# Issuing the attention stage's 24 output stores from SyncE instead of ScalarE

## The chip, the cores and the metric

The kernel runs on one core of a Trainium2 chip. The metric is the device time of one execution in microseconds (us), lower is better; of several executions the median counts.

## The reference

Chunked local attention with 8 memory keys, then two MLPs, one after the other, all in f32.

```python
q, k, v: (4, 8, 768, 64); mem_k, mem_v: (4, 8, 8, 64)     # batch, heads, tokens, head_dim
for c in range(768 // 32):                                # chunks of 32 tokens
    rows = slice(32 * c, 32 * c + 32)
    ctx  = slice(max(0, 32 * c - 16), min(768, 32 * c + 40))
    k_full, v_full = cat(mem_k, k[:, :, ctx]), cat(mem_v, v[:, :, ctx])
    a = softmax(q[:, :, rows] @ k_full.T / 8)
    attn[:, :, rows] = a @ v_full
x = attn.transpose(0, 2, 1, 3).reshape(3072, 512)
h = x @ w_in                                              # 512 x 2048
g = (a0 + a1*h + a2*h**2 + a3*h**3) / (1 + |b0|*|h| + |b1|*h**2 + 1e-6)
x = g @ w_out                                             # 2048 x 512
out = ((x @ w1) * (x @ w2)) @ w3 @ w_out2                 # 512 x 1024 twice, 1024 x 1024, 1024 x 512
```

## The kernel before

**Three stages.** The first stage, attention_and_weights, folds w3 and w_out2 into one matrix (until about 70 us of the trace), computes the attention, and splits most of the first MLP's weights into a high and a low part. The function mlps holds the two others: the first MLP, in 6 blocks of 512 tokens and 16 slots of the hidden width, and the second MLP, in 6 blocks and 8 slots. All products of the MLPs are made of three matmuls (high by high, high by low, low by high). Stage one and mlps are two blocks of the program, and no engine goes into the second before all of them have ended the first.

**The attention.** It walks over 24 tiles of 128 tokens, 6 to each batch (TPB = 6, TILES = 24); t is the number of the tile over all batches. For a tile TensorE transposes the normalised probabilities (L740), computes the scores of the tile three further on (L724, L731), transposes q and k of a later half batch in the first three batches (L712), and multiplies the probabilities by v (L753, called pv here). VectorE does the softmax (L597 to L626). ScalarE copies the transposed probabilities out of PSUM (L495), computes the exp of the tile two further on (L490), copies the product of pv out of bank 6 into one of the two buffers of xt_sb (copy_xT, L501), and then issues the DMA which stores that buffer into xT in DRAM (store_x, L507). In between it copies transposed q and k (L479, L481).

**What is ordered by hand.** Each engine runs its own list of instructions in order, and the lists are tied by semaphores. For the change these ties matter:

- copy_xT of tile t waits until the store of tile t - 2 has landed (xt_stored), since both use the same buffer;
- pv of tile t waits for its v tile, which has three buffers (v_loaded), and for copy_xT of tile t - 1 (xt_ready), since all tiles share bank 6;
- SyncE issues all loads. Its step of tile t (tile_step) issues in this order: two or three loads of q and k of a later half batch (where there is one, L297 and L304), the v loads of tile t + 3 (L326, L330), for which it waits until pv of tile t is done, and one load of a raw weight for GpSimd (L171 or L174), for which it waits until GpSimd has used the buffer before it;
- after the step of tile 15 SyncE loads the first 512 tokens of xT back as x_raw (L413). ScalarE splits off their high part after copy_xT of tiles 18 and 19 (x_his, L532), VectorE the low part after its work on tiles 19 and 20 (x_los, L668), and TensorE runs two products of the first MLP on them, inside tiles 22 and 23.

```python
            def tile_step(t):
                ...
                if t + V_BUFS < TILES:
                    sp.wait_ge(pv_done, t + 1)
                    load_v(*after(b, pos, V_BUFS))
                if t < LATE:
                    sp.wait_ge(raw_split, 2 * EARLY + t + 1)
                    load_raw(*sh.late(t + 2))
```

Of the kernel before, what the change touches and what calls it, by code (L numbers as in the profile page):

```python
# [34 lines left out]
P = 128  # L35
LINE = 1024
B, H, S, D = 4, 8, 768, 64
# [5 lines left out]
TPB = S // P  # L43
# [50 lines left out]
def after(b, pos, n=1):  # L94

    return b + (pos + n) // TPB, (pos + n) % TPB
# [116 lines left out]
def attention_and_weights(nc, q, k, v, mem_k, mem_v, w_in, w_out, w3, w_out2, poly_a, poly_b,  # L213
                          xT, bweights, weights, base, work, banks, bank, sh):
    with ExitStack() as ctx:  # L215
        x_raw, x_hi, x_lo, coef = sh.x_raw, sh.x_hi, sh.x_lo, sh.coef
        x_loaded, coef_loaded, x_hi_ready = sh.x_loaded, sh.coef_loaded, sh.x_hi_ready
        wf_stored, xt_stored = sh.wf_stored, sh.xt_stored
# [3 lines left out]
        def sem(name):  # L222
            return ctx.enter_context(nc.semaphore(name))
# [31 lines left out]
        xt_sb = Place(nc, sh.raw_at - 2 * BLK * 4, sh.raw_at)("xt_sb", [P, 2, KC, P])  # L255
# [16 lines left out]
        pv_done, xt_ready = sem("pv_done"), sem("xt_ready")  # L272
# [20 lines left out]
        def _(sp):  # L293
# [13 lines left out]
            def load_qk(hb, gs):  # L307

                for g in gs:
                    if g < Q_GROUPS:  # L310
                        if hb >= 2:
                            sp.wait_ge(turned, 1 + TURNED * (hb - 2) + PAIRS)
                        load_q(hb, g)
                    else:
                        if hb >= 2:
                            sp.wait_ge(turned, 1 + TURNED * (hb - 1))
                        load_k(hb, g - Q_GROUPS)

            def load_v(b, pos):
                u = pos % V_BUFS  # L320
                for w in range(2):
                    s = pos * P + w * WIN - LEFT
                    lo, hi = max(-s, 0), min(CTX, S - s)
                    for r0, r1 in ((lo, min(hi, CTX - MEM)), (CTX - MEM, hi)):
                        if r0 < r1:
                            sp.dma_start(v_sb[r0:r1, u, w, :].rearrange("p (h d) -> p h d", h=H),  # L326
                                         v[b, :, s + r0:s + r1, :].rearrange("h s d -> s h d"))\
                                .then_inc(v_loaded[u], 16)
                    if pos < V_BUFS:
                        sp.dma_start(v_sb[CTX:KEYS, u, w, :].rearrange("p (h d) -> p h d", h=H),  # L330
                                     mem_v[b, :, :, :].rearrange("h s d -> s h d")).then_inc(v_loaded[u], 16)
# [9 lines left out]
            def load_raw(m, w):  # L341
                sh.load_raw(sp, win_v, wout_v, m, w)

            for u in range(2):
                sp.sem_inc(wf_stored[u], 16)
                sp.sem_inc(xt_stored[u], 16)
# [47 lines left out]
            def tile_step(t):  # L394
                b, pos = t // TPB, t % TPB
                hb = t // 3 + 3 + (1 if t % 3 == 2 else 0)
                if hb < 2 * B:
                    load_qk(hb, QK_TURNS[t % 3])
                if t + V_BUFS < TILES:
                    sp.wait_ge(pv_done, t + 1)  # L400
                    load_v(*after(b, pos, V_BUFS))
                if t < LATE:
                    sp.wait_ge(raw_split, 2 * EARLY + t + 1)
                    load_raw(*sh.late(t + 2))

            for t in range(TILES):
                tile_step(t)
                if t == TILES - TPB - 3:

                    sp.wait_ge(turned, 1 + TURNED * (2 * B - 1))  # L410
                    sp.wait_ge(xt_stored[0], 16 * 3)
                    sp.wait_ge(xt_stored[1], 16 * 3)
                    sp.dma_start(x_raw[:, :, :], xT[:, :, 0:BLK]).then_inc(x_loaded, 16)  # L413
                    sp.dma_start(coef[:, 0:4], poly_a.rearrange("(o n) -> o n", o=1).broadcast_to([P, 4]))\
                        .then_inc(coef_loaded, 16)
                    sp.dma_start(coef[:, 4:6], poly_b.rearrange("(o n) -> o n", o=1).broadcast_to([P, 2]))\
                        .then_inc(coef_loaded, 16)
# [39 lines left out]
        def _(act):  # L457
            def w3_hi(i):
                act.wait_ge(w3_transposed, i + 1)
                for a in range(2):  # L460
                    nc.scalar.activation(w3t_hi[:, i % 2, a * BLK:(a + 1) * BLK], bank[2 * (i % 2) + a][:, :], ACT.Copy)\
                        .then_inc(w3_hi_ready, 1)
# [11 lines left out]
            def copy_turned(b, f, c):  # L474

                a = c % PAIRS
                act.wait_ge(turned, 2 + TURNED * (2 * b + f) + c)
                if c < PAIRS:
                    nc.scalar.activation(qT[:, f, a, :], bank[7][:, 0:HALF], ACT.Copy).then_inc(turned_copied, 1)  # L479
                else:  # L480
                    nc.scalar.activation(kT[:, f, a, :, 0:CTX], overlapping(bank[7][:, 0:SPAN]), ACT.Copy)\  # L481
                        .then_inc(turned_copied, 1)
# [4 lines left out]
            def exp(b, pos):  # L487
                act.wait_ge(centred, TPB * b + pos + 1)
                p = probs[:, pos % 2, :, :].rearrange("p h c -> p (h c)")
                nc.scalar.activation(p, p, ACT.Exp, scale=float(D) ** -0.5).then_inc(exped, 1)  # L490

            def copy_pT(b, pos):
                for half in range(2):
                    act.wait_ge(p_transposed, (TPB * b + pos) * 2 + half + 1)
                    nc.scalar.activation(pT[0:KEYS, 4 * half:4 * half + 4, :].rearrange("p h c -> p (h c)"),  # L495
                                         bank[4 + half][0:KEYS, :], ACT.Copy).then_inc(pT_ready, 1)

            def copy_xT(b, pos):
                act.wait_ge(pv_done, TPB * b + pos + 1)
                act.wait_ge(xt_stored[pos % 2], (b * (TPB // 2) + pos // 2) * 16 + 16)  # L500
                nc.scalar.activation(xt_sb[:, pos % 2, :, :].rearrange("p a c -> p (a c)"), bank[6][:, :], ACT.Copy)\  # L501
                    .then_inc(xt_ready, 1)

            def store_x(b, pos):

                act.wait_ge(xt_ready, TPB * b + pos + 2)
                act.dma_start(xT[:, :, bass.ds(b * S + pos * P, P)], xt_sb[:, pos % 2, :, :])\  # L507
                    .then_inc(xt_stored[pos % 2], 16)

            w3_hi(0)  # L510
            for n in range(JS // 2):
                act.wait_ge(wo2_loaded[n], 16)
# [16 lines left out]
            def x_his(cs):  # L529

                for c in cs:
                    nc.scalar.activation(x_hi[:, c, :], x_raw[:, c, :], ACT.Copy).then_inc(x_hi_ready, 1)  # L532

            def tile_step(b, pos, last=False):
                copy_pT(b, pos)
                if not last:
                    for c in TURNS[pos % 3][0:2]:
                        copy_turned(b + 1, pos // 3, c)
                if not last or pos < TPB - 2:
                    exp(*after(b, pos, 2))  # L540
                copy_xT(b, pos)
                if not last:
                    for c in TURNS[pos % 3][2:3]:
                        copy_turned(b + 1, pos // 3, c)
                store_x(b, pos)
                if last and pos == 0:
                    act.wait_ge(x_loaded, 16)
                    act.wait_ge(turned, 1 + TURNED * (2 * B - 1))
                if last and pos < 2:
                    x_his(range(2 * pos, 2 * pos + 2))  # L550

            with act.Fori(0, B - 1) as b:
                for pos in range(TPB):
                    tile_step(b, pos)
            for pos in range(TPB):
                tile_step(B - 1, pos, last=True)
# [726 lines left out]
```

## Time and profile before

| | |
|---|---|
| three runs | 1120.55, 1120.66 and 1123.65 us, median 1120.66 us |
| the profiled execution | 1123.65 us, span 1121.9 us |
| TensorE, VectorE, ScalarE, GpSimd busy | 97%, 63%, 52%, 15% of the span |
| granted TensorE clock, mean | 0.988 of full |
| data moved by DMA | 97.65 MB |

Busy shares are means over stages with different limits, so they say little of one stage. The attention takes some 125 us of the span (from about 74 to 199 us), the first MLP about 520, the second about 400. In a row of a timeline the first number is the start, the second the length, both in us; a bracket tells how long the engine was idle before it and what ended that. The letter q behind an engine's name (ACTq, SPq) marks what its sequencer does, issuing a DMA among others.

### The profile page before, as it was taken

Reading aid. Unit: us, or ns where it says so; the run is one execution under the profiler, and the core shown is the slowest. Engines: PE = TensorE matmul, PEld = TensorE weight load, DVE = VectorE, ACT = ScalarE, POOL = GpSimd, SP = SyncE. Lnnn points to the kernel's source line nnn. Section 1 sums busy time; section 2 is a strip of 40 time slices with the busy share of each in tenths; the row PEclk is TensorE's granted clock in tenths of the full one; section 3 lists DMA queues with packets and bytes.
Section 4 is the critical chain, followed back from the end, with each engine's and each line's share of the span. In section 5 each row is a group of like instructions: output and inputs, shape, how many; then the busy total and the mean of one; then the engine's idle time right before and its main releaser. Section 6 shows DMA issues by size and latency. Waiting matters only on the chain.

```text
span 1121.9 us, 16471 instructions
## 1 busy us (share of the span) xinstructions
PE 1088.7 (97%) x6292; PEld 896.0 (80%) x6292; DVE 706.8 (63%) x995; ACT 583.1 (52%) x960; POOL 169.0 (15%) x137
## 2 busy tenths in 40 slices
PE   8999987899999999999999999999999999999998
PEld 6877766687888888888888888888888888888886
DVE  5378875899999999999998998811212121111211
ACT  3457763677876876877787787521213122121311
POOL 4324542412122122121100100100000000000000
PEclk9999996899999999999999999999999999999999
DMA  9989994211211220121100146320202010020000
GB/s 308 265 210 248 275 259 123 75 57 48 84 56 47 71 69 28 56 85 46 56 37 0 37 150 221 116 76 1 75 0 75 0 37 37 0 75 0 37 1 38
DMA packets 138733, 97.65 MB, mean 87 GB/s; under 512 B 89548, under 2 KB 118220, under 8 KB 137676
## 3 DMA queue, kind: packets, MB, share of 16 engines
q1 hardware_dynamic: 126028, 90.92, 26.8%
q10 hardware_dynamic: 12672, 6.29, 1.9%
q8 instruction: 21, 0.34, 0.1%
q14 instruction: 12, 0.10, 0.0%
HBM read 65.74 MB, written 31.46 MB: 87 GB/s over the span
## 4 chain that ended last, share of the span: by engine, by line
PE 51%; DVE 25%; issue 4%; ACT 2%; ACTq 0%; DVEq 0%
PE banks L1199 23%; PE banks L1214 11%; PE banks L1183 9%; PE banks L205 8%; DVE nr L1102 5%; DVE nr L1099 5%; DVE nr L1106 4%; DVE g_lo L1111 3%; DVE sq L1082 3%; DVE poly L1089 3%; DVE poly L1092 1%; DVE x_lo L1068 1%; ACT y_sb L1004 1%; ACT habs L978 0%; ACT sq L981 0%
## 5 line engine op out<-in xcount | busy, mean ns | idle before, releaser
L1183 PE MATMUL banks<-g_hi,weights 128*128 128x512 f32 x768 | 253.4, 392 | 4.9 <-DVE g_lo L1111 4.8
L205 PE MATMUL banks<-x_hi,weights 128*128 128x512 f32 x768 | 253.6, 393 | 1.9 <-PEq L215 1.9
L1199 PE MATMUL banks<-x_hi,weights 128*128 128x512 f32 x768 | 244.2, 389 | 0.0
L1140 DVE TENSOR_TENSOR nr<-habs,banks 128x512 f32<-128x512 f32 x48 | 33.0, 688 | 256.7 <-ACT habs L1034 256.7
L1183 PEld LDWEIGHTS banks<-g_hi,weights 128*128 128x128 f32 x768 | 144.9, 189 | 37.7 <-DVE g_lo L1111 7.2
L205 PEld LDWEIGHTS banks<-x_hi,weights 128*128 128x128 f32 x768 | 145.7, 190 | 32.5 <-issue 2.0
L1199 PEld LDWEIGHTS banks<-x_hi,weights 128*128 128x128 f32 x768 | 144.1, 188 | 29.8
L1034 ACT ACTIVATE habs<-banks 128x512 f32<-128x512 f32 x48 | 28.6, 596 | 245.2 <-PE banks L1199 245.2
L205 PE MATMUL banks<-x_lo,weights 128*128 128x512 f32 x384 | 150.6, 392 | 0.0
L1183 PE MATMUL banks<-g_lo,weights 128*128 128x512 f32 x384 | 150.0, 391 | 0.0
L1199 PE MATMUL banks<-x_lo,weights 128*128 128x512 f32 x384 | 149.4, 389 | 0.0
L1214 PE MATMUL banks<-weights,g_hi 128*128 128x512 f32 x384 | 118.3, 389 | 0.1
L932 POOL TENSOR_TENSOR x_lo<-x_raw,x_hi 128x512 fp32r<-128x512 f32 x22 | 31.3, 1432 | 515.2 <-ACT x_hi L972 515.2
L997 ACT ACTIVATE g_hi<-nr 128x512 fp32r<-128x512 f32 x96 | 60.7, 632 | 91.5 <-DVE nr L1106 91.5
L1082 DVE SCALAR_TENSOR_TENSOR sq<-sq,bcoef,habs 128x512 f32<-128x512 f32 x96 | 73.1, 761 | 24.8 <-ACT sq L981 24.8
L989 ACT ACTIVATE rq<-sq,ln_bias 128x512 f32<-128x512 f32 x96 | 69.8, 727 | 31.4 <-DVE sq L1082 31.1
L205 PEld LDWEIGHTS banks<-x_lo,weights 128*128 128x128 f32 x384 | 72.8, 190 | 15.1
L1214 PEld LDWEIGHTS banks<-weights,g_hi 128*128 128x128 f32 x384 | 72.0, 188 | 15.4 <-DVE g_lo L1143 0.5
L1183 PEld LDWEIGHTS banks<-g_lo,weights 128*128 128x128 f32 x384 | 72.5, 189 | 14.7
L1199 PEld LDWEIGHTS banks<-x_lo,weights 128*128 128x128 f32 x384 | 72.1, 188 | 15.1
L1102 DVE SCALAR_TENSOR_TENSOR nr<-nr,rq 128x512 f32<-128x512 f32 x96 | 82.0, 854 | 3.3
L1099 DVE SCALAR_TENSOR_TENSOR nr<-sq,rq 128x512 f32<-128x512 f32 x96 | 80.9, 843 | 0.3 <-ACT rq L992 0.3
(83 smaller groups left out, 1544.0 us busy)
## 6 DMA issues: line engine op xcount, KB each, us to landing
x_raw<-x_transposed_dram SPq DMA_DIRECT2D x12, 1024.0 KB, 5.3
weights<-second_mlp_weights_dram SPq DMA_DIRECT2D x8, 1536.0 KB, 6.3
second_mlp_weights_dram<-split SPq DMA_DIRECT2D x16, 512.0 KB, 3.0
v_sb<-in_v SPq DMA_DIRECT2D x44, 160.0 KB
qk_sb<-in_q SPq DMA_DIRECT2D x24, 256.0 KB, 4.7
x_transposed_dram<-xt_sb ACTq DMA_DIRECT2D x24, 256.0 KB, 4.2
x_transposed_dram<-y_sb SPq DMA_DIRECT2D x6, 1024.0 KB, 4.9
out<-y_sb SPq DMA_DIRECT2D x5, 1024.0 KB, 4.2
```

The lines of the kernel that those rows point to most:

```text
L205: last = nc.tensor.matmul(bank[m % 4][:, :], slot[:, m, a, cols], x[:, c, :], start=c == 0 and n == 0, stop=c == KC - 1 and n == 2)
L989: nc.scalar.activation(rq[:, u, :], sq[:, u, :], ACT.Ln, scale=2.0 ** -LN_SHIFT, bias=ln_bias[:, 0:1]).then_inc(ln_ready, 1)
L997: nc.scalar.activation(g_hi[:, m % G_BUFS, :], nr[:, m % 2, :], ACT.Copy).then_inc(g_hi_ready, 1)
L1082: nc.vector.scalar_tensor_tensor(out=sq[:, u, :], in0=sq[:, u, :], scalar=bcoef[:, 1:2], in1=habs[:, u, :], op0=ALU.mult, op1=ALU.add).the ...
L1089: nc.vector.tensor_tensor(out=poly[:, u, :], in0=poly[:, u, :], in1=h[:, :], op=ALU.mult)\
L1099: nc.vector.scalar_tensor_tensor(out=nr[:, u, :], in0=sq[:, u, :], scalar=Q_ONE, in1=rq[:, u, :], op0=ALU.add, op1=ALU.mult).then_inc(e_re ...
L1102: nc.vector.scalar_tensor_tensor(out=nr[:, u, :], in0=nr[:, u, :], scalar=-2.0, in1=rq[:, u, :], op0=ALU.add, op1=ALU.mult).then_inc(r1_re ...
L1106: nc.vector.scalar_tensor_tensor(out=nr[:, u, :], in0=poly[:, u, :], scalar=ncoef[:, 0:1], in1=nr[:, u, :], op0=ALU.add, op1=ALU.mult).the ...
L1111: nc.vector.tensor_tensor(out=g_lo[:, m % G_BUFS, :], in0=nr[:, m % 2, :], in1=f32(g_hi[:, m % G_BUFS, :]), op=ALU.subtract).then_inc(g_lo ...
L1183: last = nc.tensor.matmul(bank[4 + c][:, :], slot[:, m, a, cols], g[:, m % G_BUFS, :], start=m == 0 and n == 0, stop=m == SLOTS - 1 and n ...
L1199: last = nc.tensor.matmul(bank[2 * (j % 2) + w][:, :], bslot[:, j, 2 + 2 * w + a, cols], x[:, c, :], start=c == 0 and n == 0, stop=c == KC ...
L1214: last = nc.tensor.matmul(bank[4 + t][:, :], c[:, j % G_BUFS, cols], bslot[:, j, a, :], start=j == 0 and n == 0, stop=j == JS - 1 and n == 2)
```

## The change

The store of a tile is issued by SyncE instead of ScalarE. The wait for the tile's copy (xt_ready) goes with it. It stands in SyncE's step of the same tile, behind the v loads and ahead of the raw weight load. The bytes, the buffers and the semaphores stay as they were, and so do all other instructions.

```diff
@@ block.sync @@
+            def store_x(b, pos):
+                sp.wait_ge(xt_ready, TPB * b + pos + 2)
+                sp.dma_start(xT[:, :, bass.ds(b * S + pos * P, P)], xt_sb[:, pos % 2, :, :])\
+                    .then_inc(xt_stored[pos % 2], 16)
...
                 if t + V_BUFS < TILES:
                     sp.wait_ge(pv_done, t + 1)
                     load_v(*after(b, pos, V_BUFS))
+                store_x(b, pos)
                 if t < LATE:
                     sp.wait_ge(raw_split, 2 * EARLY + t + 1)
                     load_raw(*sh.late(t + 2))
@@ block.scalar @@
-            def store_x(b, pos):
-
-                act.wait_ge(xt_ready, TPB * b + pos + 2)
-                act.dma_start(xT[:, :, bass.ds(b * S + pos * P, P)], xt_sb[:, pos % 2, :, :])\
-                    .then_inc(xt_stored[pos % 2], 16)
...
                 if not last:
                     for c in TURNS[pos % 3][2:3]:
                         copy_turned(b + 1, pos // 3, c)
-                store_x(b, pos)
                 if last and pos == 0:
```

## Rows read from the trace of the kernel before

**Rows 1.** Busy time by stretch; then clock, DMA share of 16 engines, GB/s.

```profile
84.00:157.00 73.00, 66.34 (x1214) 54.31 (x1213) 60.96 (x88) 52.50 (x98) 35.96 (x32) 0.98 1.06 261
157.00:199.20 42.20, 31.35 (x439) 25.53 (x438) 24.79 (x38) 18.81 (x32) 12.65 (x12) 0.80 0.56 151
199.20:543.40 344.20, 339.30 (x1476) 278.70 (x1476) 334.56 (x444) 252.38 (x404) 67.67 (x48) 0.99 0.18 60
```

**Rows 2.** DMA queues from 0 to 60 us: packets, MB, share of 16 engines.

```profile
q1 hardware_dynamic: 26560, 17.08, 96.7%
```

**Rows 3.** DMA queues from 84 to 157 us, and one group of issues.

```profile
q1 hardware_dynamic: 50894, 15.19, 87.7%
q10 hardware_dynamic: 7747, 3.84, 17.7%
...
x_transposed_dram<-xt_sb ACTq DMA_DIRECT2D x15, 256.0 KB, 4.2
```

**Rows 4.** Timeline of SyncE's queue, steps of tiles 0, 8, 11, 13, 15, 16.

```profile
77.28 0.38 SPq L171 DMA_DIRECT2D raw_w<-in_moe_w_in  x1
...
122.92 0.98 SPq L171 DMA_DIRECT2D raw_w<-in_moe_w_in  x1
...
140.99 0.36 SPq L174 DMA_DIRECT2D raw_w<-in_moe_w_out  x1
...
151.14 0.35 SPq L174 DMA_DIRECT2D raw_w<-in_moe_w_out  x1
...
157.60 0.62 SPq L413 DMA_DIRECT2D x_raw<-x_transposed_dram  x1
...
165.30 0.51 SPq L330 DMA_DIRECT2D v_sb<-in_mem_v  x1
165.86 0.40 SPq L171 DMA_DIRECT2D raw_w<-in_moe_w_in  x1
```

**Rows 5.** Timeline of ScalarE, around the copies of tiles 2, 10, 13, 15, 18.

```profile
85.40 0.59 ACT L501 ACTIVATE xt_sb<-banks 128x512 f32<-128x512 f32 x1
...
119.77 0.58 ACTq L507 DMA_DIRECT2D x_transposed_dram<-xt_sb  x1
120.47 1.08 ACT L495 ACTIVATE pT<-banks 96x512 f32<-96x512 f32 x2 [0.47 <-PE banks L740]
...
123.83 0.59 ACT L501 ACTIVATE xt_sb<-banks 128x512 f32<-128x512 f32 x1
...
138.45 0.59 ACT L501 ACTIVATE xt_sb<-banks 128x512 f32<-128x512 f32 x1
...
150.71 0.59 ACT L501 ACTIVATE xt_sb<-banks 128x512 f32<-128x512 f32 x1
...
164.28 0.60 ACT L501 ACTIVATE xt_sb<-banks 128x512 f32<-128x512 f32 x1 [0.60 <-PE banks L753]
```

**Rows 6.** Timeline of ScalarE around the copy of tile 19.

```profile
170.53 0.84 ACT L490 ACTIVATE probs<-probs 128x768 f32<-128x768 f32 x1 [1.94 <-DVE probs L606]
172.40 0.60 ACT L501 ACTIVATE xt_sb<-banks 128x512 f32<-128x512 f32 x1 [1.02 <-PE banks L753]
173.03 0.56 ACTq L507 DMA_DIRECT2D x_transposed_dram<-xt_sb  x1
173.63 1.15 ACT L532 ACTIVATE x_hi<-x_raw 128x512 fp32r<-128x512 f32 x2 [0.64 <-ACT xt_sb L501]
```

**Rows 7.** Timeline of VectorE, the low part after tile 19.

```profile
167.22 0.69 DVE L668 TENSOR_TENSOR x_lo<-x_raw,x_hi 128x512 fp32r<-128x512 f32 x1 [2.48 <-ACT x_hi L532]
```

**Rows 8.** Timeline of TensorE, pv of tiles 14 and 19.

```profile
143.87 1.15 PE L753 MATMUL banks<-pT,v_sb 96*64 96x64 f32 x32 [1.80 <-DMA v_sb<-in_mem_v]
...
170.38 1.97 PE L753 MATMUL banks<-pT,v_sb 96*64 96x64 f32 x32 [3.36 <-DMA v_sb<-in_mem_v]
```

**Rows 9.** Timeline of ScalarE, end of the stage.

```profile
197.97 0.54 ACTq L507 DMA_DIRECT2D x_transposed_dram<-xt_sb  x1
```

## The prediction

> **What bounds the kernel now.** I read the busy times by stretch first. In the first MLP VectorE is busy 334.56 of 344.20 us and the second MLP is a plain run of matmuls; neither touches the code changed. The change lives between 74 and 199 us, and whatever date the attention ends at moves both MLPs by as much, because all engines enter them together. In 84 to 157 us no compute engine is full, but the 16 DMA engines show a share of 1.06 at 261 GB/s [rows 1]. So the attention's middle is a matter of DMA.
>
> The queues of that stretch show SyncE's queue (q1) with 87.7% of the 16 engines and ScalarE's (q10), which carries nothing but the stores, with 17.7%. Fifteen stores were issued there, so one costs 0.177 x 73 / 15 = 0.86 us of all engines; it lands 4.2 us after its issue (median) [rows 3].
>
> Then SyncE's timeline against ScalarE's. The raw weight load ends SyncE's step of a tile, and its start is where the new store would stand. The step of tile 0 gets there at 77.28, tile 8 at 122.92, tile 11 at 140.99, tile 13 at 151.14, tile 16 at 165.86 [rows 4]: 88.6 us for 16 steps, 5.5 each. The copies on ScalarE, from tile 2 at 85.40 to tile 13 at 138.45, come every 4.8 us [rows 5]. The compute runs faster than its loads, lives on the three v buffers, and SyncE falls further behind. At tile 14 the cushion is used up: pv waits 1.80 us for a v load; at tile 19 it waits 3.36 us [rows 8]. After that SyncE has little left to load. Thus the loads date pv of tile 19, and from there a compute chain runs to the end: copy of tile 19 (172.40), x_hi (173.63), x_lo on VectorE, and VectorE's work on the next tiles behind it, which waits its turn as it does at the x_lo before (167.22) [rows 6, 7].
>
> **What the change removes.** On ScalarE 24 issues of about 0.56 us. In mid stage they lie on its path: the store of tile 9 ends at 120.35 and the next copy of probabilities starts at 120.47 [rows 5]. Up to tile 18 that gain is worth nothing as long as loads set the pace. Behind that the issue after the copy of tile 19 stands between copy and x_hi [rows 6]; I count it below. At the very end the issue of the last store, 0.54 us at 197.97 [rows 9], is made by SyncE as soon as the copy is done: zero, as both engines wait for the same copy, then issue.
>
> **What it adds: a shorter leash.** SyncE comes to the store of tile t behind all its loads, and copy_xT of t + 2 must wait for it to land. With the dates of SyncE's steps plus 4.2 us against the present copy: tile 2: 81.5 against 85.40, free; tile 10: 127.1 against 123.83, 3.3 late; tile 13: 145.2 against 138.45, 6.8 late; tile 15: 155.3 against 150.71, 4.6 late [rows 3 to 5]. Between tile 2 (3.9 early) and tile 10 the sign turns at about tile 6, and from there on ScalarE waits at the copy in nearly every tile, the copies behind it on ScalarE (probabilities, q and k) wait too, and TensorE and VectorE with them. The compute, which was ahead, is now tied two tiles behind SyncE. By itself this costs nothing while SyncE sets the date of tile 19 anyway, as long as the leash doesn't hold back SyncE in turn. It doesn't: SyncE's v loads in the step of tile t wait for pv of t, which is done by 4.2 + 4.8 = 9.0 us after the store of t - 3 (landing, then one copy to the next), while SyncE is there three steps less its own v loads later, some 13 us. What counts is the last coupling.
>
> **The coupling at tile 18.** SyncE reaches the store of tile 16 at 165.86, held up by the 1 MB load of x_raw issued at 157.60 [rows 4]. What is issued right there lands slower than the median: the last v load, issued at 165.30, lets pv go at 170.38, 5.1 us later [rows 4, 8]. So copy 18 starts at about 165.86 + 5.1 = 171.0 instead of 164.28 [rows 5]. Then, with the lengths of the present rows: copy 0.60, x_hi 0.58 (half of 1.15), then VectorE from x_lo to the exp on ScalarE as now (167.22 to 170.53, 3.31), exp 0.84, copy 19 0.60. That gives x_hi of tile 19 at 171.0 + 0.6 + 0.6 + 3.3 + 0.8 + 0.6 = 176.9, with the 0.56 us of the removed issue already out of it, against 173.63 [rows 5 to 7]. The chain to the end starts 3.3 us later. With the median landing of 4.2 it would be 2.4; with 6 us 4.2.
>
> **Does SyncE itself get later?** The bytes are the same, but one queue must now carry what two carried. Below nothing: two stores fewer (0 to 16 instead of 0 to 18) are in front of the v loads by 165.86, 2 x 0.86 = 1.7 us less. This can hardly be cashed: the copies of tiles 14 and 15 come so close behind SyncE's short steps 14 and 15 that it would wait for them. So 0 is the lower end. Above: if the stores added in full to q1's own time, 17 x 0.86 = 14.6 us. In between: in 0 to 60 us q1 works alone, and full, at 96.7% [rows 2]; together the two make 105.4% [rows 3]. Carrying 1.054 at 0.967 makes steps 9% longer, 88.6 x 0.09 = 8.0, less 1.7, so 6.3 us. The packets of 0 to 60 us are larger (17.08 MB in 26560, 643 bytes, against 15.19 MB in 50894, 298 bytes), so that stretch does not prove that two queues are needed to reach 105%. I take 4 us, between 0 and 6.3 to 8.
>
> The profile here says that two queues together hold a higher share (105.4% against 96.7%) [rows 2, 3]. The Trainium skill, "DMA: Bandwidth & Descriptors", section "Issuing engines are not separate DMA queues", says that DMAs of all issuing engines run on the same 16 DMA engines, so several issuers save only sequencer time. By that rule the 4 us are 0 and the sum ends with the 3.3 us of the leash, 1124.0; that is rival A below.
>
> **Sum.** 3.3 + 4 = 7.3 us, against the profiled execution's own 1123.65 us (span 1121.9 and 1.75 around it) 1131.0. That execution is the longest of three; measured on the median of 1120.66 I forecast 1128.0.
>
> **Rivals.** (A) No measurable change: stores land in 4.2 us or less and SyncE loses nothing, so 2.4 to 3.3 us, 1123.1 to 1124.0. For it: equal bytes; the leash binds off the path up to tile 17. Against it: 165.86 is a late date for a store whose buffer is wanted at 164.28. A measurement of this kernel tells about 0.3%, 3.4 us, from nothing.
>
> (B) TensorE's clock. Tiles now wait in mid stage. Where pv waited 1.80 and 3.36 us the clock afterwards fell from 2.4 to 1.2 GHz for a while: pv took 1.97 us against 1.15 [rows 8], and the stretch 157 to 199.2 has 0.80 against 0.98 before [rows 1]. TensorE is busy 66.34 of 73 us there [rows 1], 4.4 in a tile of 4.8; times 1.7 that is 7.5, 2 us more than SyncE's 5.5. In six tiles of the twelve that wait this is 12 us on top: 1140. For it: from tile 6 waits of 1 us and more. Against it: the waits in a tile are only the difference between 4.8 and 5.5 us, spread over it, and a late TensorE lets SyncE catch up. If q1 takes the full 14.6 us, the sum is 17.9: 1138.6, the same region.
>
> (C) Faster. The queue for loads alone moved 17.08 MB in its first 60 us, 285 GB/s, against 261 with both [rows 1, 2]. If a single queue also keeps that here, the 88.6 us shrink by 8.4%, 7.5 us, and ScalarE, rid of its issues, can follow (4.8 less 0.35 to 0.56 is under SyncE's 5.0 a step). Then 3.3 - 7.5 = -4.2: 1116.5. It decides from 6.7 us saved on. Against it: those first packets are twice as large, which alone can account for the higher rate.
>
> **Chances.** The forecast (3.4 to 12 us slower) 0.56; A 0.20; B, with a full price on q1, 0.15; C 0.09. Range: from just below A to the beginning of B, 1119 to 1142, leaving out about 0.1 on either side. Slower by over 0.3%: 0.56 + 0.15 = 0.71; the same 0.21; faster 0.08.
>
> **What would show it.** In the trace after, q10 is gone, and ScalarE's copy of xt_sb waits for a DMA (x_transposed_dram from xt_sb) from about tile 6 on, and no longer TensorE for v. The copy of tile 18 is at 171 or later instead of 164.28; x_hi of tile 19 near 181 instead of 173.63; the MLP starts near 206 instead of 199.2. SyncE at the raw load of tile 16 near 170 would confirm the 4 us; 166 would mean the queue costs nothing, 180 that it costs in full. I am wrong if copies don't wait for stores, if v loads land earlier than now, or if the granted clock between 84 and 157 us is well below 0.98. Both MLPs should last as before, 922.7 us together.

## The result and the profile after

| | before | after |
|---|---|---|
| median of 5 runs | 1121.70 us (1120.55 to 1123.65) | 1127.89 us (1126.63 to 1129.42) |
| ratio | | 1.0052, 95% interval 1.0038 to 1.0065 |
| profiled execution | 1123.65 us, span 1121.9 | 1123.61 us, span 1121.8 |

The change makes the kernel 0.52% slower, 5.8 us. A second timing gave 1.0060 (1.0042 to 1.0078), 6.7 us. Yet the two profiled executions are equal to 0.1 us. That of before is slower than most of its kind, that of after faster than the five timed. So a trace must here be read for dates inside it, not for its length.

The stretch and the queues of 84 to 157 us in the trace of after (the columns as in [rows 1, 3]):

```profile
84.00:157.00 73.00, 62.84 (x1100) 50.95 (x1100) 57.35 (x82) 48.05 (x92) 34.39 (x29) 0.95 1.02 249
```

```profile
q1 hardware_dynamic: 56098, 18.10, 101.8%
...
x_transposed_dram<-xt_sb SPq DMA_DIRECT2D x13, 256.0 KB, 2.9
```

The queue q10 is gone, and q1 alone now holds a share of 101.8%. In the same 73 us 13 stores were issued where 15 were [rows 3], and all transfers together moved 249 GB/s against 261 [rows 1]. A store lands sooner after its issue, 2.9 us against 4.2.

ScalarE's waits between 64 and 200 us (total, times, longest), and its timeline from the copy of tile 17 on:

```profile
ACT xt_sb L507 <- DMA x_transposed_dram<-xt_sb: 15.8, 10, 3.4
```

```profile
103.33 0.60 ACT L507 ACTIVATE xt_sb<-banks 128x512 f32<-128x512 f32 x1 [1.67 <-DMA x_transposed_dram<-xt_sb]
...
164.27 0.59 ACT L507 ACTIVATE xt_sb<-banks 128x512 f32<-128x512 f32 x1
...
170.47 0.60 ACT L507 ACTIVATE xt_sb<-banks 128x512 f32<-128x512 f32 x1 [3.37 <-DMA x_transposed_dram<-xt_sb]
170.96 1.14 ACT L532 ACTIVATE x_hi<-x_raw 128x512 fp32r<-128x512 f32 x2
...
175.64 0.84 ACT L496 ACTIVATE probs<-probs 128x768 f32<-128x768 f32 x1 [2.58 <-DVE probs L605]
176.39 0.58 ACT L507 ACTIVATE xt_sb<-banks 128x512 f32<-128x512 f32 x1
176.87 1.14 ACT L532 ACTIVATE x_hi<-x_raw 128x512 fp32r<-128x512 f32 x2
```

Ten copies wait for a store, 15.8 us in all. The first is that of tile 6 (103.33). The copy of tile 18 (170.47) waits for the store of tile 16, and the high part of x behind tile 19 starts at 176.87 instead of 173.63 [rows 6]. SyncE's queue shows the other side:

```profile
160.46 0.63 SPq L419 DMA_DIRECT2D x_raw<-x_transposed_dram  x1
...
166.37 0.57 SPq L346 DMA_DIRECT2D x_transposed_dram<-xt_sb  x1
166.98 0.99 SPq L171 DMA_DIRECT2D raw_w<-in_moe_w_in  x1
```

The 1 MB load of x_raw is issued 2.9 us later than before [rows 4], the store of tile 16 at 166.37, and it lets the copy go 4.1 us later. From 176.87 to the first MLP it takes 22.2 us; in the trace of before it took 25.6 (173.63 to 199.20). That is how 3.2 us were lost and 3.4 won back in this one execution. The next section shows with what.

### The profile page after: what moved, and what is told of

The parts are those of the page before. It is cut to its first block, busy times and chain, and to the rows that moved or that the text cites. A ratio compares the mean times of both kernels' runs of the same rounds, so it can differ in the third digit from the quotient of the medians.

```text
span 1121.8 us, 16430 instructions
## 1 busy us (share of the span) xinstructions
PE 1083.9 (97%) x6292; PEld 892.7 (80%) x6292; DVE 706.5 (63%) x995; ACT 581.9 (52%) x960; POOL 169.7 (15%) x137
## 4 chain that ended last, share of the span: by engine, by line
PE 51%; DVE 25%; issue 4%; ACT 2%; ACTq 0%; DVEq 0%
PE banks L1198 23%; PE banks L1213 11%; PE banks L1182 9%; PE banks L205 8%; DVE nr L1101 5%; DVE nr L1098 5%; DVE nr L1105 4%; DVE g_lo L1110 3%; DVE sq L1081 3%; DVE poly L1088 3%; DVE poly L1091 1%; DVE x_lo L1067 1%; ACT y_sb L1003 1%; ACT sq L980 0%; ACT poly L981 0%
```

## The experiments

All ratios are against the kernel before on the same chip, in 5 rounds. "Leash" is the tie of a copy to a store that SyncE issues late. The leash theory puts the loss down to it, the queue theory to one queue carrying less than two, the issue-time theory to the time that SyncE spends on an issue. One profile was taken of each kernel below, and these of its dates are compared (us): the issue of the raw load of tile 16 on SyncE (in e9 and e10, where SyncE has none, the store; a dash where it has neither there), pv of tile 19, x_hi of tile 19, the start of the first MLP, and the granted clock from 180 to 190 us.

| kernel | ratio (95%) | SyncE tile 16 | pv 19 | x_hi 19 | MLP starts | clock |
|---|---|---|---|---|---|---|
| before, first profile | | 165.86 | 170.38 | 173.63 | 199.20 | 0.50 |
| before again (b1) | 1.0001 (0.9987, 1.0014) | 163.37 | 168.04 | 171.82 | 195.95 | 0.73 |
| after, first profile | 1.0052 (1.0038, 1.0065) | 166.98 | 173.21 | 176.87 | 199.06 | 0.92 |
| after again (a1) | 1.0060 (1.0042, 1.0078) | 170.50 | 175.84 | 179.40 | 201.32 | 0.82 |
| e1 six buffers | 1.0031 (1.0017, 1.0045) | 171.93 | 174.43 | 177.45 | 202.58 | 0.67 |
| e2 store ahead of v | 1.0042 (1.0025, 1.0060) | 169.47 | 173.22 | 176.24 | 200.53 | 0.84 |
| e3 leash alone | 1.0020 (1.0009, 1.0031) | 166.13 | 173.47 | 178.27 | 199.38 | 0.82 |
| e4 leash on tile 18 | 1.0019 (1.0006, 1.0033) | 164.22 | 172.35 | 176.76 | 200.17 | 0.69 |
| e5 small loads on SyncE | 1.0067 (1.0052, 1.0081) | 172.11 | 175.05 | 178.68 | 203.26 | 0.67 |
| e6 raw loads put off | 1.0013 (1.0004, 1.0022) | - | 165.51 | 169.26 | 196.79 | 0.58 |
| e7 SyncE delayed, no DMA | 1.0078 (1.0063, 1.0093) | 172.45 | 176.87 | 180.12 | 203.87 | 0.67 |
| e8 raw loads by GpSimd | 0.9992 (0.9978, 1.0007) | - | 167.68 | 171.44 | 193.95 | 0.83 |
| e9 the same, on after | 1.0037 (1.0021, 1.0053) | 166.88 | 175.54 | 178.56 | 199.46 | 0.91 |
| e10 e1 and e9 together | 1.0041 (1.0028, 1.0053) | 168.27 | 171.58 | 174.02 | 200.67 | 0.58 |

**a1 and b1, both kernels again.**

> The changed kernel again, for a second profile and a second timing. Leash theory: slower than before by 4 to 8 us, copy of tile 18 waits 2 to 4 us for the store of tile 16 and the low part of x starts 3 us later than in the kernel before. The profile of the first execution of the change spanned 1121.8 us although its median was 1127.9; if TensorE's clock decides from execution to execution how much of the 3 us survives, this profile's span is nearer 1126 and its granted clock between 157 and 199 us is lower than 0.92.

> The kernel before again, as a control and for a second profile. Ratio 0.999 to 1.001. Its first profiled execution was 3 us over its median, with TensorE at 1.2 GHz from 180 to 190 us and 25.6 us from the high part of x after tile 19 to the first MLP. If the granted clock there is what makes the executions differ, a profile of a span near 1119 has these two at about 0.8 or more and 22 us, with v-load dates as in the first profile.

The second profile of after has its x_hi at 179.40, that of before at 171.82. Taking both pairs, the change moves that date by 5.4 us (178.1 against 172.7), and SyncE's date at tile 16 by 4.1 (168.7 against 164.6). The start of the MLP moves by only 2.6 us in these pairs (200.2 against 197.6), less than the 5.8 to 6.7 us of the timings; two profiles of each kernel are too few to place the rest. The rest of the stage takes 20.9 to 27.5 us over the 14 profiles, and the low values go with a high granted clock (busy times and clock from 180 to 190 us; before, b1, after, a1):

```profile
180.00:190.00 10.00, 8.45 (x55) 7.22 (x56) 7.10 (x15) 3.81 (x6) 0.00 (x0) 0.50 0.27 73
```

```profile
180.00:190.00 10.00, 9.23 (x97) 7.80 (x95) 5.05 (x13) 4.26 (x7) 0.00 (x0) 0.73 0.14 41
```

```profile
180.00:190.00 10.00, 7.76 (x122) 6.38 (x121) 9.71 (x20) 5.43 (x9) 0.72 (x1) 0.92 0.41 111
```

```profile
180.00:190.00 10.00, 7.21 (x116) 5.75 (x115) 9.74 (x14) 5.57 (x10) 4.39 (x4) 0.82 0.68 174
```

With 0.50 (all at 1.2 GHz) the tail took 25.6 us, with 0.73 24.1, with 0.92 22.2 and 0.82 21.9. TensorE was idle ahead of pv of tile 19 in each of them; whether it is back at 2.4 GHz when the two products of the MLP come differs from execution to execution. This goes some way to explain the scatter of 3 us in the times of one kernel: in the 25 timed executions of before that stand beside a1, time and mean granted clock are correlated by -0.72, but in the six of a1 by 0.08. Two expectations were missed. The second profile of before had a clock of 0.73 and a tail of 24.1 us, not 0.8 and 22, and its dates were earlier. That of after had 0.92 between 157 and 199 us, no less than the first; it was longer because its dates came later. From the start of the MLP to the end it is 922.6 to 922.8 us in every profile.

**e3 and e4, the leash alone.** The stores stay on ScalarE; a copy waits for the v tile that stands right ahead of the store in the changed kernel, on every tile (e3) or on tile 18 only (e4).

```diff
                 act.wait_ge(xt_stored[pos % 2], (b * (TPB // 2) + pos // 2) * 16 + 16)
+                if not last or pos < TPB - 1:                 # e4: if last and pos == 0
+                    nb, np = after(b, pos)
+                    act.wait_ge(v_loaded[np % V_BUFS], v_count(nb, np))
```

> The kernel before, stores on ScalarE's own queue, with one thing added: the copy of tile t waits for the v tile t + 1 to have landed, the transfer that stands right ahead of the store of t - 2 in the changed kernel. Leash theory: slower as the change is or a little more, since ScalarE also keeps its issues: ratio 1.004 to 1.008. Queue theory: no change, 0.999 to 1.001.

> The kernel before with one wait added, for tile 18 only: its copy waits until the v tile 19 has landed. The prediction's reckoning (only the last coupling counts): slower by as much as with the leash on every tile, 2 to 3.5 us, ratio 1.002 to 1.003, copy of tile 18 at 170 us. Rival (the waits in mid stage cost too, by TensorE's clock and by delaying SyncE): under half of it, 1.000 to 1.001.

The ratios are 1.0020 and 1.0019, about 2.2 us each. In e4 the copy of tile 18 waits 6.4 us for v of tile 19:

```profile
168.81 0.60 ACT L503 ACTIVATE xt_sb<-banks 128x512 f32<-128x512 f32 x1 [6.39 <-DMA v_sb<-in_mem_v]
```

In e3 the copies fall behind as in the changed kernel (tile 13 at 144.67, in after 144.39, in before 138.45), and yet it costs no more than e4. So the waits of the tiles up to 17 add nothing that was measured, within the intervals of about 0.1% either way. The cost is less than half of the loss, so the expectation of the leash theory for e3 (1.004 or more) failed. The v load only stands in for the store: the copy of tile 18 comes at 169.91 and 168.81 here, at 170.47 and 173.10 with the change, so the real leash may cost somewhat more.

**e1, no leash.** Six buffers instead of two in the first three batches; the four new ones lie in the place of weight slot 9. One expression of the edit:

```diff
-        xt_sb[:, pos % 2, :, :]
+        xt_sb[:, pos % 2, :, :] if last or pos < 2 else xt_more[:, pos - 2, :, :]
```

> The change with four more xt buffers in the first three batches (weight slot 9's place, free until its split), so that no copy waits for a store before tile 20, and stores still on SyncE's queue. Leash theory: the whole loss goes away, ratio 0.998 to 1.001 against before, copy of tile 18 at 162 to 166 us. Queue theory (one queue carries less than two): the loss stays, ratio 1.003 to 1.006, and v loads land later than before.

No copy waits for a store, and 0.31% stays. SyncE comes to tile 16 at 171.93, 6.1 us later than in the first profile of before and 8.6 later than in b1. What this delays is the load of x_raw more than v: x_hi of tile 18 on ScalarE waits 6.6 us for it, the copy of the probabilities stands behind it in ScalarE's list, and pv of tile 19 on TensorE behind that. Both rows, and the queue in 84 to 157 us:

```profile
172.17 1.15 ACT L549 ACTIVATE x_hi<-x_raw 128x512 fp32r<-128x512 f32 x2 [6.62 <-DMA x_raw<-x_transposed_dram]
...
174.43 1.97 PE L769 MATMUL banks<-pT,v_sb 96*64 96x64 f32 x32 [6.80 <-ACT pT L512]
```

```profile
q1 hardware_dynamic: 55237, 17.81, 99.8%
```

GpSimd waits 10.3 us for the borrowed place, but its low part of x is done at 186.2 and TensorE comes to the products at 190.6, so that this wait is off the path. So far this looked like the queue theory: 99.8% for one queue, 105.4% for two. It needed a test of its own.

**e5 and e7, SyncE's time without the bytes.** The kernel before; each step of SyncE gets, where the store would be, two loads of 16 pieces of 16 bytes (e5), or 16 increments of a semaphore that nobody waits for (e7).

```diff
+                for n in (2 * t, 2 * t + 1):                  # e5
+                    sp.dma_start(tiny[0:16, n, :], poly_a.rearrange("(o n) -> o n", o=1)
+                                 .broadcast_to([16, 4])).then_inc(tiny_loaded, 16)
...
+                for n in range(16):                           # e7
+                    sp.sem_inc(idle_count, 1)
                 if t < LATE:
                     sp.wait_ge(raw_split, 2 * EARLY + t + 1)
```

> The kernel before with two loads of 16 pieces of 16 bytes added to every step of SyncE where the changed kernel has its store; the stores stay on ScalarE's queue. It takes SyncE's issue time (0.5 to 0.7 us a step, against 0.55 for a store) and nearly no bytes. If the later v loads come from SyncE's issue time: raw load of tile 16 at 169 to 172 instead of 165.9 and ratio 1.002 to 1.004. If they come from what one queue carries: the added issues only take from SyncE's waiting for room, raw load at 166 to 167, ratio 0.999 to 1.001.

> The kernel before with 16 semaphore increments and no transfer added to every step of SyncE, where the changed kernel has its store. If SyncE's time alone is what the small loads cost (issue-time theory), each step gets later by what the 16 take, less than the 0.88 us of the two small loads if an increment takes under 0.05 us: raw load of tile 16 at 168 to 172, ratio 1.002 to 1.006. If it was the place that a transfer takes in the queue, however small: raw load as before (163.4 and 165.9 in two profiles), ratio 0.999 to 1.001.

Both are slower than the change itself, 1.0067 and 1.0078, though no store has moved. SyncE's queue in e7 around one such place, and the stretch of 84 to 157 us:

```profile
108.48 0.31 SPq L331 DMA_DIRECT2D v_sb<-in_mem_v  x1
109.79 0.36 SPq L174 DMA_DIRECT2D raw_w<-in_moe_w_out  x1
```

```profile
84.00:157.00 73.00, 63.81 (x1167) 52.06 (x1165) 60.76 (x83) 50.50 (x93) 31.62 (x30) 0.98 1.00 244
```

The gap ahead of the raw load grows from 0.04 to 1.00 us (108.79 to 109.79), 0.95 us a step. With both queues in use, the DMA share falls from 1.06 to 1.00 and the raw load of tile 16 comes at 172.45. A share of 1.00 is thus no sign that one queue carries less than two: it falls as far when SyncE issues later. Nor is 96.7% what one queue holds, since q1 alone has 101.8% in the changed kernel. The queue theory in the form that I gave it fell here; SyncE's time alone can make loads late by as much. The changed kernel asks 0.83 us a step of it: 0.55 and a gap of 0.04 for the store, and the transfer right behind the store takes longer to issue, 0.63 us (median of 17) against 0.40 and 0.36 for the two kinds of raw load before.

Not all of it comes through. From the raw load of tile 0 to that of tile 16 it takes 88.6 and 84.5 us in the two profiles of before, 94.1 in e7 and 89.7 and 92.3 in after. So some 7.5 of 15.2 us arrive in e7, and 4.5 of 13.3 with the change (estimates, from the means); the rest is made up by shorter issues and waits of SyncE elsewhere.

**e8 and e9, SyncE relieved.** GpSimd issues the 20 raw loads of the attention itself, behind the split which frees the buffer, on before (e8) and on after (e9).

```diff
@@ block.sync, tile_step @@
-                if t < LATE:
-                    sp.wait_ge(raw_split, 2 * EARLY + t + 1)
-                    load_raw(*sh.late(t + 2))
...
@@ block.gpsimd @@
                 sh.split_weights(...)
+                pool.wait_ge(raw_split, 2 * EARLY + t + 1)
+                sh.load_raw(pool, win_v, wout_v, *sh.late(t + 2), sh.raw_pool)
```

> The kernel before, but GpSimd issues the 20 raw weight loads of the attention itself, each right after the split that frees the buffer, so SyncE is rid of 0.43 us of issues a step. Issue-time theory: v loads of tile 19 land 3 us earlier or more, the x_raw load too, faster by 1 to 4 us (0.997 to 0.999), part of it given back as TensorE is left waiting for VectorE at 1.2 GHz. Rival (16 DMA engines are full): no earlier v loads, ratio 0.999 to 1.001; slower if GpSimd's transfers crowd out SyncE's.

> The changed kernel (stores on SyncE) with the same 20 raw loads issued by GpSimd. SyncE then has one transfer more and one less a step than in the kernel before. Issue-time theory: the later v loads are gone, copies wait for stores less, and most of the 0.5 to 0.6% goes: ratio 0.999 to 1.002 against before. Queue-capacity theory: SyncE's queue carries the same bytes as before the change, so the same is expected, but with the share of all queues staying near 1.05; leash theory alone (stores land late whatever issues them): 1.002 to 1.004.

The stretch of 84 to 157 us in e8, all engines (columns as in [rows 1]):

```profile
84.00:157.00 73.00, 66.71 (x1262) 54.53 (x1262) 69.78 (x91) 53.76 (x101) 55.58 (x54) 1.00 1.09 278
```

e8 moves more than any other kernel, 1.09 and 278 GB/s, though b1 has 1.08 and 269 without any change: the DMA engines had a little room left, not much. SyncE is earlier, its load of x_raw at 154.11 against 157.60 and 156.15 in the two profiles of before; but x_hi of tile 19 comes at 171.44, no earlier than in b1 (171.82). The copies come every 4.9 us, the pace that they had in before, so compute is probably the next bound. 0.9992 (0.9978 to 1.0007) is no gain that was measured: the 1 to 4 us that the issue-time theory promised did not come, and the ratio is also what full DMA engines would give. e9 stays at 1.0037, against an expected 0.999 to 1.002: nine copies still wait for stores (15.0 us), and now SyncE waits ten times for pv (9.8 us). The leash works in both directions there.

**e10, both costs removed.** The edits of e1 and e9 together.

> The changed kernel with both of its costs taken away: six xt buffers in the first three batches (no copy waits for a store before tile 20) and the 20 raw loads issued by GpSimd (SyncE has no more issues a step than before). If leash and SyncE's issue time are the whole loss of 0.5 to 0.6%, nothing of it is left: ratio 0.998 to 1.001. If a third cost exists (stores and loads in one queue), 1.002 to 1.004.

1.0041, where nothing was expected to be left. But the edit does not take SyncE's cost away. A transfer right behind a store takes longer to issue here too; the same load of q in e10 and in e8:

```profile
143.78 0.54 SPq L354 DMA_DIRECT2D x_transposed_dram<-xt_more  x1
144.37 0.63 SPq L305 DMA_DIRECT2D qk_sb<-in_q  x1
```

```profile
138.98 0.39 SPq L298 DMA_DIRECT2D qk_sb<-in_q  x1
```

All 17 transfers behind a store take 0.62 to 0.84 us, while such loads of q took 0.38 to 0.43 at their quickest in e8 and before. So a step of e10 asks not 0.16 us more of SyncE than in before (0.59 for a store with its gap against 0.43 for a raw load) but up to 0.4, an estimate from these rows. SyncE is at tile 16's store at 168.27, 3.7 us behind the mean of the two profiles of before, nearly as late as in the changed kernel. e9 and e10 are therefore no test of what remains once SyncE is relieved, and e10 reads as a second case without a leash, 0.41% beside the 0.31% of e1. A third cost, stores and loads in one queue, was named ahead of the run with 1.002 to 1.004; no run excludes it. In place of the leash GpSimd waited 16.2 us for the borrowed buffers, but its low part of x was done at 185.2 and TensorE came to it at 188.1.

There is no fixed price for SyncE's time. By the added time of a step it is 0.8% for each us in e7 (0.78 for 0.95) and e5 (0.67 for 0.88), 0.4 in e1 (0.31 for 0.83), and 0.6 to 0.7 with the change, which has the leash besides.

**e2, the store ahead of the v loads.**

```diff
@@ block.sync, tile_step @@
+                store_x(b, pos)
                 if t + V_BUFS < TILES:
                     sp.wait_ge(pv_done, t + 1)
                     load_v(*after(b, pos, V_BUFS))
-                store_x(b, pos)
```

> The change with the store put ahead of the step's v loads instead of behind them: the leash is about 3 to 4 us shorter (for tile 16, 162.3 instead of 166.4). Leash theory: copy of tile 18 at 165.5 to 166.5 instead of 170.5, and most of the loss goes: ratio 1.000 to 1.002. Queue theory: unchanged, 1.004 to 1.006.

The store of tile 16 in SyncE's queue of e2, and the copy of tile 18 that waits for it in ScalarE's timeline:

```profile
163.50 0.59 SPq L346 DMA_DIRECT2D x_transposed_dram<-xt_sb  x1
```

```profile
170.48 0.60 ACT L507 ACTIVATE xt_sb<-banks 128x512 f32<-128x512 f32 x1 [2.39 <-DMA x_transposed_dram<-xt_sb]
```

The store of tile 16 goes out at 163.50, 2.9 us earlier than in after, and lands at 170.4 all the same: nearly 7 us, right behind the 1 MB of x_raw (issued at 161.68). Moving the issue doesn't help where the queue in front of it is long. The copy of tile 18, expected at 165.5 to 166.5, came at 170.48, and the ratio of 1.0042 lies inside the interval of the change. So this run doesn't separate the theories: it did not shorten the leash at tile 18.

**e6, fewer loads ahead of tile 19, on before.** The raw loads of steps 13 to 15 go to steps 16 to 19.

```diff
@@ block.sync, tile_step @@
-                if t < LATE:
-                    sp.wait_ge(raw_split, 2 * EARLY + t + 1)
-                    load_raw(*sh.late(t + 2))
+                for n in {16: (13,), 17: (14, 15), 18: (16, 17), 19: (18, 19)}.get(
+                        t, () if t in (13, 14, 15) or t >= LATE else (t,)):
+                    sp.wait_ge(raw_split, 2 * EARLY + n + 1)
+                    load_raw(*sh.late(n + 2))
```

GpSimd's low part of x moves ahead of its split of step 18 with it.

> The kernel before, but the raw weight loads of steps 13, 14 and 15 are issued in the steps 16 to 19 instead, behind the v loads of tile 19, and GpSimd makes its parts of the low x before its last two splits. If v loads date the end of the attention: 0.75 MB less ahead of them, 2.5 us, pv of tile 19 at 168 instead of 170.4, faster by 1.5 to 3 us, ratio 0.997 to 0.999. If not: 1.000.

pv of tile 19 came at 165.51 and x_hi at 169.26, the earliest of all, and earlier than expected; but the kernel was 0.13% slower, where 0.1 to 0.3% faster was expected. The tail took 27.5 us at a clock of 0.58. So nothing is gained by earlier v loads alone in the kernel before. Why the tail grew by more than the profile's clock in other runs would give was not tried.

## Why the prediction was right, step by step

The forecast was 1128.0 us, 7.3 over the median then known; measured were 1127.89, 5.8 to 6.7 us over before in the two timings. The sign and the size hold. That the times agree to 0.1 us is luck: the median of before had moved from 1120.66 to 1121.70 meanwhile, one term was too large, and the other had its size for a wrong reason. Of its steps:

- **The leash** held as worked out: copies wait from tile 6 on, 103.33 the first; copy of tile 18 at 171.0 forecast, 170.47 and 173.10 found; x_hi at 176.9 without any delay of SyncE, 176.87 found in the profile where SyncE was 1.1 us late at the raw load (0.5 at the place of the store). The exact 176.87 is in part chance, since the store landed 4.0 us after its issue and not 5.1. The term of 3.3 us in the time looks oversized: the stand-in for the leash measured 2.2 (1.0 to 3.5). That only tile 18 counts, e3 and e4 together bear out.
- **SyncE later by 4 us**: 4.1 us between the means of two profiles each (raw load of tile 16), with 2.5 to 3.5 us between two profiles of one kernel; 7.3 in e1. The size was fair, the reason was not. The prediction priced what one queue carries against two, 96.7% against 105.4%, but q1 alone reached 101.8% in the trace of after, and e7 shows a larger delay with two queues and no added byte. The time that a store's issue takes on SyncE has no term in it: 0.56 us was taken off ScalarE and nothing put on SyncE. In the runs a third to a half of such time came through.
- **The removed issues on ScalarE** were put at nothing in mid stage; no run tests them alone, and nothing contradicts it. The gain of 0.56 us behind tile 19 can be seen (x_hi follows the copy at 0.48 us, against 1.23 in [rows 6]).
- **The start of the MLP near 206** was missed in both profiles, 199.06 and 201.32. I took the tail of the first profile, 25.6 us, as fixed; it is 20.9 to 27.5. That profile was also 3 us longer than the median. From the median of 1127.89, less 1.8 around the span and 922.7 for the MLPs, the start would be 203.4 in a typical execution (an estimate).
- **Rival B** was half there: the clock between 84 and 157 us fell to 0.95 and 0.91, which the prediction had named as a sign against it, yet the 12 us that it put on this did not come. e3 and e4 cost the same, but at 0.98 and 1.00 they don't price so low a clock; what the slower clock in mid stage costs was not tested.
- **The page's rule.** The Trainium skill ("DMA: Bandwidth & Descriptors", section "Issuing engines are not separate DMA queues") says that several issuers save only the sequencer's time, which is usually small relative to the DMA itself. The runs agree with the first half: one queue reached a share of 101.8%, where two had 105.4% in the same stretch of before [rows 3]. They don't contradict the second, 0.55 us to issue a store that lands 2.9 us after. The prediction went wrong in reading from it that SyncE loses nothing: the sequencer's time that two issuers save is what the change gives up.

**Shown:** SyncE's time alone, without bytes, is enough for losses of this size (e5, e7). With no copy waiting for a store, 0.31% stays (e1). A leash on the v load costs 0.20% at tile 18 alone and no more on every tile (e3, e4). **Argued:** that these two make up the change. 0.20 and 0.31 add up to 0.51 of 0.52 to 0.60, but e5 and e7 lose as much as the change or more with no leash at all, and the intervals of about 0.13% either way leave other splits open. **Open:** the split itself, since no run took SyncE's cost away with the stores on it; whether stores and loads in one queue cost anything beyond that; and the price of the clock in mid stage.

## What to carry to other kernels

Before moving a transfer to the queue that "only does DMA", add up that queue's own timeline: if its issues stand end to end, added time there can land on whatever its last load feeds (here a third to a half of it did). A DMA share near 1 does not tell whether the engines or the issuer set the pace; a delay of the issuer without bytes helps to tell. A store in an in-order list also inherits every wait ahead of it, so ask what its buffer's next writer must now wait for, and check a 0.3% effect on dates and timings of several executions rather than on one profile.

## What the runs showed of the hardware

- Sixteen semaphore increments on SyncE added 0.95 us to a gap of 0.04, about 60 ns each (e7).
- A transfer issued right behind a store of xt took 0.63 us to issue (median of the raw loads of either kind in after), against 0.40 (L171) and 0.36 (L174) in before. In e2, where the raw load is not behind a store, it is 0.39 and 0.36 again, and in e9 and e10 the loads of q, k and v that follow a store take 0.63 (median).
- The share of the DMA engines reached 1.09 at 278 GB/s with three queues in use (e8), with the same transfers that gave 1.06 at 261 and 1.08 at 269 with two (before, b1). One queue alone reached 101.8% (after).
- A 256 KB store issued 1.8 us after the 1 MB load of x_raw landed 6.9 us after its issue (e2), against a median of 2.9 in after and 4.2 in before.
